# The third stage of an attention and feed-forward kernel in spans of 1024 and 896 tokens, all by Strassen's products

## The reference

```python
p_packed = sm_attn(p, k, v)
out = sm_attn(q, p_packed, p_packed)
x = out.transpose(0, 2, 1, 3).reshape(4608, 512)
h = x @ w_in                                   # 512 -> 1024
solu = h * softmax(h)
ln = (solu - mean) / sqrt(var + 1e-6) * g_ln
x = ln @ w_out                                 # 1024 -> 512
h = max(x @ w1, x @ w2, x @ w3)                # 512 -> 768 each
return h @ w_out2                              # 768 -> 512
```

## Time and profile before

| | |
|---|---|
| time, median of 3 runs | 1015.54 us (1014.46 to 1017.72) |
| profiled execution | 1014.56 us, span 1012.8 us |
| granted PE clock | 1.00 of full speed |
| PE busy | 990.8 us (98%) |
| DVE, ACT, POOL busy | 587.8, 357.4, 269.6 us |
| third stage, group matmuls | 1512 and 216, 512 columns each |
| third stage, output matmuls | 648, 512 columns each |

### The profile page before, as it was taken

The page is one execution under the profiler, slowest core; times in us unless marked ns, Lnnn a source line. Parts: engine busy times, 40 slices in busy tenths (PEclk is TensorE's granted clock), DMA queues, the critical chain, the costliest instruction groups (busy, mean ns, idle before and its releaser), DMA issues.

```text
span 1012.8 us, 14951 instructions
## 1 busy us (share of the span) xinstructions
PE 990.8 (98%) x6026; PEld 795.1 (79%) x6026; DVE 587.8 (58%) x960; ACT 357.4 (35%) x585; POOL 269.6 (27%) x229
## 2 busy tenths in 40 slices
PE   6999999999999999999999999999999999999998
PEld 5656668887887887878888888888888888888887
DVE  2788889765775666574565625673466635553121
ACT  5877753343342442343221422224122332123111
POOL 0368762629949992600000000000000000000000
PEclk9999999999999999999999999999999999999999
DMA  9999717426636481236654345543554536532341
GB/s 300 389 305 312 290 66 260 169 93 247 250 149 231 187 319 45 102 115 253 235 216 163 140 163 211 183 181 127 185 206 166 193 111 218 176 126 94 120 160 42
DMA packets 49764, 189.85 MB, mean 187 GB/s; under 512 B 9888, under 2 KB 9888, under 8 KB 39328
## 3 DMA queue, kind: packets, MB, share of 16 engines
q1 hardware_dynamic: 43472, 153.89, 42.6%
q0 software_dynamic: 6224, 35.00, 9.3%
HBM read 141.30 MB, written 47.58 MB: 186 GB/s over the span
## 4 chain that ended last, share of the span: by engine, by line
PE 86%; DVE 5%; issue 3%; POOL 2%; ACT 2%; DMA 1%; SPq 0%; ACTq 0%; POOLq 0%; DVEq 0%
PE ps L1191 29%; PE ps L801 28%; PE ps L1223 15%; PE ps L1214 5%; PE ps L1093 3%; PE ps L911 1%; PE ps L815 1%; DVE h_lo L1619 1%; PE ps L1011 1%; DVE spot L1932 1%; DVE spot L1923 1%; PE ps L960 1%; PE ps L861 1%; DMA p_raw<-in_p_dram 1%; POOL m_odd L708 1%
## 5 line engine op out<-in xcount | busy, mean ns | idle before, releaser
L1191 PE MATMUL ps<-ys,slot 128*128 128x512 f32 x1512 | 345.7, 390 | 0.5
L1191 PEld LDWEIGHTS ps<-ys,slot 128*128 128x128 f32 x1512 | 283.2, 188 | 62.5 <-ACT spot L1268 3.9
L1923 DVE TENSOR_TENSOR spot<-ps,spot 128x512 f32<-128x512 f32 x108 | 74.3, 688 | 104.2 <-PE ps L1191 75.1
L1268 ACT ACTIVATE spot<-ps 128x512 f32<-128x512 f32 x90 | 52.8, 596 | 207.9 <-PE ps L1191 196.8
L801 PE MATMUL ps<-ln_lo,w_out_s_hi 128*128 128x512 f32 x280 | 109.2, 390 | 0.0
L801 PE MATMUL ps<-ln_hi,w_out_s_lo 128*128 128x512 f32 x280 | 109.0, 389 | 0.0
L801 PE MATMUL ps<-ln_hi,w_out_s_hi 128*128 128x512 f32 x280 | 109.0, 389 | 0.0
L1223 PE MATMUL ps<-w_out_s_lo,h_hi 128*128 128x512 f32 x216 | 84.0, 389 | 0.0
L1223 PE MATMUL ps<-w_out_s_hi,h_hi 128*128 128x512 f32 x216 | 84.0, 389 | 0.0
L1223 PE MATMUL ps<-w_out_s_hi,h_lo 128*128 128x512 f32 x216 | 84.0, 389 | 0.0
L1432 ACT ACTIVATE u<-ps,neg_max 128x1024 f32<-128x1024 f32 x36 | 40.2, 1117 | 109.9 <-DVE neg_max L1781 109.9
(11 more groups left out here) (164 smaller groups left out, 1496.0 us busy)
## 6 DMA issues: line engine op xcount, KB each, us to landing
slot<-w_operands SPq DMA_DIRECT2D x36, 1792.0 KB, 7.3
w_operands<-stage POOLq DMA_DIRECT2D x18, 1024.0 KB, 4.9
v_raw<-in_v_dram SPq DMA_DIRECT2D x8, 1152.0 KB, 6.7
q_raw<-in_q_dram SPq DMA_DIRECT2D x32, 288.0 KB, 5.5
y_features<-yst SPq DMA_DIRECT2D x9, 1024.0 KB, 4.7
y_raw<-y_features SPq DMA_DIRECT2D x9, 1024.0 KB, 5.3
out_dram<-spot SPq DMA_DIRECT2D x36, 256.0 KB, 2.1
slot<-w_operands SPq DMA_DIRECT2D x9, 1024.0 KB, 5.0
```

What stands on the lines that cost most here:

```text
L1191: last = pe.matmul(ps[:, group_bank(g, k), :], w[:, a - 1, i, kk, :], ys[:, b, j, kk, :], start=n < 4 and kk == 0 and e == 0, stop=kk == K ...
L1268: return act.activation(dst, src, ACT.Copy)
L1923: dve.tensor_tensor(dst[:, :], a, b, op).then_inc(ready, 1)
```

## The change

The third stage goes over the tokens in five spans: one of 2 x 512 tokens and four of 2 x 448 (HALVES). All use Strassen's products; the plain rest, with its functions (plain_group, load_last_y, hi_last_y, copy_plain, hi_plain), is gone. In a span of 896 tokens the group matmuls, the copies, sums, maxima and splits work on 448 columns, and there are 7 output tiles; the fourth of them lies across both halves of h2, so the wait for all of a triple's low parts stands ahead of tile 3 instead of tile 4. The order of the work on each queue stays. Every span loads 7 operands a group, 45 slots in all. In the second stage, POOL splits and stores A22, A11 and A12 only, not A21, so that the first of its two stores for each group has three operands instead of four. y_raw has the same place and size with its middle dimensions merged. The core of the diff:

```diff
-FOUR = TOKENS // (2 * BLK)
-TPF = 2 * TPB
+HALVES = (512, 448, 448, 448, 448)
+SPANS = len(HALVES)
+SPAN_TILES = tuple(2 * n // P for n in HALVES)
+FIRST_TILE = tuple(itertools.accumulate((0, *SPAN_TILES[:-1])))
...
-        return FILLS * g + FILLS if g < GROUPS * FOUR else FILLS * GROUPS * FOUR + 2 * (g - GROUPS * FOUR) + 2
+        return FILLS * g + FILLS
...
             def load_y(t, kk):
-                src = y_dram.rearrange("p (h k) n -> p k h n", h=2)[:, kk, :, 2 * BLK * t:2 * BLK * (t + 1)]
-                sp.dma_start(y_raw[:, :, :, :].rearrange("p h c n -> p h (c n)"), src).then_inc(y_loaded, 16)
-
-            def load_last_y():
-                sp.dma_start(y_raw[:, :, :, :].rearrange("p h c n -> p (h c) n"), y_dram[:, :, 2 * BLK * FOUR:TOKENS])\
-                    .then_inc(y_loaded, 16)
+                cols = slice(FIRST_TILE[t] * P, (FIRST_TILE[t] + SPAN_TILES[t]) * P)
+                src = y_dram.rearrange("p (h k) n -> p k h n", h=2)[:, kk, :, cols]
+                sp.dma_start(y_raw[:, :, 0:2 * HALVES[t]], src).then_inc(y_loaded, 16)
 
             def load_slot(g):
-                t, s = divmod(g, GROUPS)
                 if g >= RING:
 
                     sp.wait_ge(g_filled, group_end(g - RING))
-                if t < FOUR:
-                    dst, src = slots[g % RING][:, :, :, :, :], w_dram[s][:, 1:8]
-                else:
-                    dst, src = slots[g % RING][:, 0:4, :, :, :], w_dram[s][:, 0:4]
-                sp.dma_start(dst.rearrange("p o e k n -> p (o e k n)").bitcast(F32),
-                             src.rearrange("p o e k n -> p (o e k n)")).then_inc(slot_loaded[g % RING], 16)
+                sp.dma_start(slots[g % RING][:, :, :, :, :].rearrange("p o e k n -> p (o e k n)").bitcast(F32),
+                             w_dram[g % GROUPS][:, 1:8].rearrange("p o e k n -> p (o e k n)")).then_inc(slot_loaded[g % RING], 16)
...
-            for t in range(FOUR):
-
-                sp.wait_ge(y_split, 2 * Y_PARTS * (t + 1))
-                if t < FOUR - 1:
+            for t in range(SPANS):
+                if t < SPANS - 1:
+
+                    sp.wait_ge(y_split, 2 * Y_PARTS * (t + 1))
                     load_y(t + 1, 0)
-                else:
-                    load_last_y()
                 for s in range(GROUPS):
-                    load_slot(GROUPS * t + s + RING)
-                for j in range(TPF):
-                    store_out(TPF * t + j)
-                    if j == 1 and t < FOUR - 1:
+                    if GROUPS * t + s + RING < GROUPS * SPANS:
+                        load_slot(GROUPS * t + s + RING)
+                for j in range(SPAN_TILES[t]):
+                    store_out(FIRST_TILE[t] + j)
+                    if j == 1 and t < SPANS - 1:
 
                         sp.wait_ge(y_split, 2 * Y_PARTS * (t + 1) + Y_PARTS)
                         load_y(t + 1, 1)
-            for s in range(GROUPS - RING):
-                load_slot(GROUPS * FOUR + s + RING)
-            for j in range(TPB):
-                store_out(TPF * FOUR + j)
...
-                pool.tensor_scalar(stage[:, 0:4, 0, :, :], raw, 1.0, None, ALU.mult).then_inc(weight_hi, 1)
+                plain = raw[:, 1:4]
+                pool.tensor_scalar(stage[:, 1:4, 0, :, :], plain, 1.0, None, ALU.mult).then_inc(weight_hi, 1)
                 pool.wait_ge(weight_hi, n + 1)
-                pool.tensor_tensor(stage[:, 0:4, 1, :, :], raw, stage[:, 0:4, 0, :, :].bitcast(F32), ALU.subtract)\
+                pool.tensor_tensor(stage[:, 1:4, 1, :, :], plain, stage[:, 1:4, 0, :, :].bitcast(F32), ALU.subtract)\
                     .then_inc(weight_split, 1)
                 wait_alone(pool, weight_split, n + 1)
-                pool.dma_start(w_dram[s][:, 0:4], stage[:, 0:4, :, :, :].bitcast(F32)).then_inc(w_stored[0], 16)
+                pool.dma_start(w_dram[s][:, 1:4], stage[:, 1:4, :, :, :].bitcast(F32)).then_inc(w_stored[0], 16)
...
+                w, cols = slots[g % RING], slice(0, HALVES[t])
...
-                    pe.wait_ge(o2_copied, TPF * (t - 1) + TPB * (s + 1))
+                    pe.wait_ge(o2_copied, FIRST_TILE[t - 1] + min(TPB * (s + 1), SPAN_TILES[t - 1]))
...
-                            last = pe.matmul(ps[:, group_bank(g, k), :], w[:, a - 1, i, kk, :], ys[:, b, j, kk, :],
+                            last = pe.matmul(ps[:, group_bank(g, k), cols], w[:, a - 1, i, kk, :], ys[:, b, j, kk, cols],
...
-            def plain_group(g):
-                s = g - GROUPS * FOUR
...
+                pe.wait_ge(h2_split, base + 4 * (MH - 1))
+                pe.wait_ge(c12_ready, GROUPS * (t + 1) - 1)
+                down2(t, 0, early)
+                down2(t, 1, early)
+
+                pe.wait_ge(h2_split, base + 4 * (MH - 1) + 2)
+                down2(t, 0, late)
+                down2(t, 1, late)
+                for j in range(2, SPAN_TILES[t]):
+                    if j == HALVES[t] // P:
+
+                        pe.wait_ge(h2_split, base + 4 * MH)
+                    down2(t, j, early + late)
+
+            for t in range(SPANS):
                 for s in range(GROUPS):
                     group(GROUPS * t + s)
-                outputs(t, TPF)
-            for s in range(GROUPS):
-                plain_group(GROUPS * FOUR + s)
-            outputs(FOUR, TPB)
+                outputs(t)
...
             def hi_y(t, kk):
-                half = 2 * t + kk
+                half, n = 2 * t + kk, HALVES[t]
...
+                copy(ys[:, B11:B21 + 1, 0, kk, 0:n], y_raw[:, :, 0:n]).then_inc(y_hi, 1)
...
-            def hi_last_y():
-                act.wait_ge(y_loaded, 16 * 2 * FOUR + 16)
-                act.wait_ge(g_filled, group_end(GROUPS * FOUR - 1))
-                for h, b in enumerate((B11, B21)):
-                    copy(ys[:, b, 0, :, :], y_raw[:, h, :, :]).then_inc(y_hi, 1)
...
-                copy(firsts[g % 2][:, :], ps[:, group_bank(g, 0), :]).then_inc(first_copied, 1)
+                n = HALVES[g // GROUPS]
+                copy(firsts[g % 2][:, 0:n], ps[:, group_bank(g, 0), 0:n]).then_inc(first_copied, 1)
...
+                    copy(h2[0][:, MH * m + i, c * n:(c + 1) * n], best[m][c][:, 0:n]).then_inc(h2_hi, 1)
...
             def lo_y(t, kk):
-                half = 2 * t + kk
+                half, n = 2 * t + kk, HALVES[t]
+                turned = [x[:, 0:n] for x in turn]
...
-                        dve.wait_ge(out_stored[j], 16 * TPF * t // 2)
+                        dve.wait_ge(out_stored[j], 16 * ((FIRST_TILE[t] - j + 1) // 2))
...
-            def plain_group(g):
-                q, w = divmod(g, 3)
...
             lo_y(0, 0)
             lo_y(0, 1)
-            for t in range(FOUR):
+            for t in range(SPANS):
                 for s in range(GROUPS):
                     group(GROUPS * t + s)
-                if t < FOUR - 1:
+                if t < SPANS - 1:
                     lo_y(t + 1, 0)
                     lo_y(t + 1, 1)
-                else:
-                    lo_last_y()
-            for s in range(GROUPS):
-                if s % 3:
-                    plain_group(GROUPS * FOUR + s)
 
```

More of the change, by code:

```diff
@@ L12 @@
+import itertools
 import concourse.bass as bass
@@ L1194, in group, with down2 @@
                     last.then_inc(g_filled, 1)
-            def plain_group(g):
-                s = g - GROUPS * FOUR
[L1198 to L1203, removed]
-                else:
[L1206 to L1220, removed]
+            def down2(t, j, chunks):
                 for c in chunks:
                     for e, (a, z) in enumerate(PASSES):
-                        last = pe.matmul(ps[:, out_bank(n), :], h2[a][:, c, j * P:(j + 1) * P],
+                        last = pe.matmul(ps[:, out_bank(t, j), :], h2[a][:, c, j * P:(j + 1) * P],
                                          w_out2_s[z][:, c, :], start=(c == 0 and e == 0),
@@ L1227, in down2, with outputs @@
                     last.then_inc(o2_filled, 1)
-            def outputs(t, tiles):
+            def outputs(t):
                 early = [c for c in range(K2) if c % MH < MH - 1]
                 late = [c for c in range(K2) if c % MH == MH - 1]
-                parts = 4 if t < FOUR else 2
                 base = 4 * MH * t
[L1235 to L1254, removed]
-            for t in range(FOUR):
+                pe.wait_ge(h2_split, base + 4 * (MH - 1))
[10 more added lines that the diff above has]
+            for t in range(SPANS):
                 for s in range(GROUPS):
                     group(GROUPS * t + s)
-                outputs(t, TPF)
-            for s in range(GROUPS):
-                plain_group(GROUPS * FOUR + s)
-            outputs(FOUR, TPB)
+                outputs(t)
         @block.scalar
@@ L1922, in add @@
-            def add(dst, a, b, ready, op=ALU.add):
-                dve.tensor_tensor(dst[:, :], a, b, op).then_inc(ready, 1)
+                low(5, T4, turned[1])
+                low(6, T3, turned[0])
             def group(g):
```

(39 more changed lines are left out.)

113 lines of the change are left out of this document (34 added, 79 removed).

## The result

The changed kernel took 1017.48 us (median of 10 runs, 1016.35 to 1018.20) against 1014.91 (10 runs, 1014.15 to 1017.72): ratio 1.0021, 95% interval 1.0013 to 1.0029. It is slower by 2.1 us (1.3 to 2.9), clear of no change, though by less than 0.3%. The forecast was 2.2 us faster. The number lies in the range that I gave (1010.0 to 1019.0) but outside that of the likeliest case (1012.0 to 1015.5), and the sign was wrong.

A forecast was written before the change was run, and what follows sets the result against it. Third stage bound by PE's matmuls plus two stops a span: 119.05 + 4 x (104.16 + 2 x 0.45) = 539.3 us against 541.47, so 1015.54 - 2.16 = 1013.4 us; range 1010.0 to 1019.0.

The forecast's parts named there:

- the likeliest case: Whole kernel: the forecast within 199.3 to 201.7 ns a matmul, chance 0.45, giving 1012.0 to 1015.5 us.
- What bounds the kernel: Third stage: PE's matmuls, 118.32 us of a 119.05 us full span, plus two stops losing 0.73 us.
- the cost of a matmul of 448 columns: Group matmuls of the narrow spans: 186.7 ns streaming plus a fixed 13.3 ns, taken as 200.0 ns.
- rival (b): Group matmuls: narrower ones cost more than a fixed extra, up to 207.1 ns, 6.8 us slower; chance 0.09.
- the sign of being wrong: Group matmuls: an interval off 200 ns by more than 1.7, or a ninth kind of wait, would refute the prediction.
- The stop: PE waits for DVE and ACT twice a span: each stop grows from 0.365 to 0.45 us in narrow spans.
- Rival (a): Group matmuls: the whole 226.67 ns scales with columns, 198.3 ns at 448, 4.3 us less; chance 0.30.
- (c): Group matmuls: the weight load sets the pace, interval stays 226.67 ns, 34.5 us more; chance 0.03.
- (d): Stops: the DVE and ACT chain doesn't shrink, 1.19 us each, 3.7 us more; chance 0.08 together with (e).
- (e): A cover at a span's edge or a slot fails, each microsecond counting four times; chance 0.08 with (d).
- the slots: 45 operand loads: each lands in 7.3 us with 16.8 us between issue and use, so it hides.
- A21: Second stage: leaving out its split and store cuts POOL's work by a quarter and changes the time by nothing.

The follow-up runs named there:

- before_early: The kernel before with ACT's copy_first of the next group moved ahead of the last high part of a triple; 1012.43 us, ratio 0.9973.
- spans384: The changed kernel with half spans of 512, 512, 512, 384, 384 columns instead of 512 and four of 448; 1013.04 us, ratio 0.9980 to the kernel before.
- after: The changed kernel itself in its first profile; median 1017.48 us, ratio 1.0021 to the kernel before; the profiled execution took 1017.0 us.
- after_again: The changed kernel without any edit, run once more with another profile; 1016.90 us.
- a21_back: The changed kernel with A21 split and stored again in the second stage; 1016.69 us, ratio 1.0014 to the kernel before.

## Why the prediction was wrong

*What bounds the kernel* was right: the third stage is the sum of its matmuls and two stops a span. before_early shows the stops to be worth what was read from the table, 0.73 us a span (119.05 to 118.32).

*The step that failed is the cost of a matmul of 448 columns*: "I take 200.0", because "a part of the extra that belongs to the instruction, not to its columns, is the ordinary case". It is 202.67 ns, inside the bounds (198.3 to 207.1) and beyond the 201.7 from which rival (b) said that the saving is gone; it is also off 200 by more than the 1.7 ns that the prediction named as the sign of being wrong. But (b)'s picture, a slope between narrow and wide, isn't what happens either: 384 columns have 173.3 ns, just the fixed 13.3 that I assumed. 448 is one of the widths at which the extra is larger. Nothing in the trace of before could show that; the bounds were right and the choice inside them, on which the sign hung, rested on what is ordinary. It deserved an even chance rather than 0.45 to 0.09. That the time still fell in the range confirms nothing: the range was 9 us wide.

The sum again with what was measured, for the third stage of the two profiled executions:

| term | forecast, us | measured, us |
|---|---|---|
| spacing of 1512 matmuls at 448, against 200.0 ns | 0 | +4.0 |
| stops, 8 narrow ones | 3.6 | 2.8 |
| one triple in the slow pattern | 0 | +0.4 |
| all, against before | -2.2 | +1.5 |

Together -2.2 + 4.0 - 0.8 + 0.4 = 1.4, within rounding of the 1.5. The stop is (105.86 - 28.56 - 76.61) / 2 = 0.345 us instead of 0.45. The way it was computed holds: with a spacing of 202.67 the cover shrinks by 31 x 0.024 = 0.744, as much as the chain (0.74), so it stays at about 0.365. (At 384 columns the same working gives 0.54, and spans384 shows 1.1 us for two.)

In the three traces with correct widths and all stops (after, after_again, a21_back) the third stage is 1.0 to 1.8 us longer than before, while the runs say 2.1 (1.3 to 2.9). More triples in the slow pattern in other runs would fill that, at 0.4 us each and eight places in a run; I didn't see those runs from inside, so this stays open.

*Rival (a)*, all in proportion to the columns: out. *(c)*, the weight load as pace: out at 448, though it may be what sets the floor of 111 ns at 224 to 192 columns. The Trainium skill, "TensorE: Matmul & The Clock Gate", "Back-to-back issue gap", gives 81 ns at 128 columns and 131 at 512 for pairs of load and matmul. Here 512 columns have 226.6 ns and 192 have 111, so neither its level nor its slope is that of these fp32r matmuls. By the same section of the Trainium skill the isolated gap is columns / 2.4 + 2.5 ns. Between 384 and 512 columns that slope is what the table shows; the extra is too small. *(d)*: out, DVE operations of 448 elements last about 0.62 us and ACT copies 0.54. *(e)*, the edges, and the slots: no wait of PE there in any trace, even at 384 columns, where a group is 7.3 us long and a slot takes as long to land. *A21*: no effect in any trace, as said.

## What to carry to other kernels

When a loop is cut into narrower pieces, the spacing at the new width is the number on which all hangs, and it can't be had from the spacing at another width: one kernel in which the width varies from group to group gives the whole table in a single trace. Of several splits with the same total of columns take the one whose widths have the smallest extra. And a stop that repeats can be worth more than the gain of such a split: two moved lines on ACT's queue brought 2.8 us where the whole change cost 2.

## What the runs showed of the hardware

- fp32r matmuls of 128x128 weights, each with its own load, follow each other at columns / 2.4 GHz plus 13.3 ns at 512, 496 and 384 columns, but plus 16.0 or 20.0 at 448 and 16.6 at 480. At 448 the starts alternate in a cycle of five (202, 203, 202, 199, 207 ns) or stay at 206 to 207.
- Which of the two patterns holds is set at an interruption and kept until the next: a stop of 0.3 us, or a group of another width, can change it. Operands shifted by 64 columns leave the fast pattern as it is (105.9 us a span), and a quarter of the load takes 0.5 ns off.
- From 224 to 192 columns the spacing stays at 111 to 112 ns with 128 loaded columns. At a granted clock of 0.50, 128 and 64 columns have 212.7 and 212.4 ns.
